# Score products that alternate between upper and lower rows, and r*k on GpSimd, in a linear-attention and two-MoE kernel

## Chip, cores and metric

One core of one Trainium2 chip. The metric is the device time of one execution in microseconds (us), lower is better. The engines are called TensorE (PE in the profile; PEld are its weight loads), VectorE (DVE), ScalarE (ACT), GpSimd (POOL) and SyncE (SP, which issues most DMAs). All tensors here are float32.

## The reference

The first of three layers is the one that the change touches: a linear attention with a per-element decay w, for 4 batches, 8 heads, 768 positions and heads of 48.

```
for t in range(S):
    cur = u * k_t (outer) v_t
    y[t] = r_t @ (state + cur)
    state = w_t * state + k_t (outer) v_t
```

Its output, as 3072 rows of 384, goes through a mixture of 8 experts with one expert per row (cosine logits, softmax gate, ReLU MLP 384-1024-384), and then through a second mixture in which each expert takes at most 384 rows, chosen greedily by score. These two layers are untouched.

## The kernel before, in words

The attention runs in 24 chunks of 128 positions (`NT = 24`), six to a batch (`C = 6`), all 8 heads of a chunk at once. The heads lie in pairs: head 2a in the lower 64 partitions and head 2a+1 in the upper 64 of block a, for a = 0 to 3 (`PR = 4`, `HP = 64`). Each engine has its own loop over the iterations t, and handles chunks at fixed distances from t; semaphores tie the loops together. One iteration moves every chunk on by one step.

- **VectorE**, iteration t: `take_x(t-1)` (L717), which adds the diagonal term to y; the two scans of the decays of chunk t+2, `scan_after` (L663) and `scan_before` (L673), with a small reciprocal (L666) between; `mask_scores(t+1)` (two instructions, L698); `add_state(t)` (L707, or L710 where t is a multiple of 6; none where t+1 is); `decay_k(t+2)` (L682), k times decay; `product(t+2)` (L690), r times k; and in two iterations of three some five tiny routing instructions (`choose`, `place`). `take_x` adds a term from SBUF to one from PSUM, and the mask is the only SBUF input of L698; the scans, L682 and L690 read two SBUF inputs each.
- **GpSimd**, iteration t: `decay_r(t+2)` (L467), r times decay, which waits for `scan_before(t+2)`, and from iteration 6 on `scatter(t-6)` (L478), an indirect DMA of finished rows.
- **ScalarE**, iteration t, in this order: `check(t+1)` (L507), `diag_evac(t+1)` (L539), `x_evac(t-1)` (L527), four heads of `weigh_v(t)` (L518), `y_evac(t)` (L533), `diag_out(t+1)` (L545), the other four heads, `k_evac(t+1)` (L554), `carry(t)` (L575), and in every third iteration `tokens` (L583).
- **TensorE**, iteration t: `score(t+1)` (L822), `diag_sums(t+1)` (L855), `update(t)` (L888), `x_forward(t-1)` (L829), `diag_back(t+1)` (L861), `values(t)` (L842 for the carried state, L846), `logits(t-1)` (L874), sometimes `counts`, `k_transposes(t+1)` (L918), `x_back(t)` (L926). Where t+1 is a multiple of 6 less one, that is in iterations 4, 10, 16 and 22, `scored` (L901) stands in the place of `k_transposes`, and the iteration after it has `scored_back` (L909) in the place of `update`. Where t is a multiple of 6 there is no L842.
- **SyncE** loads the chunk t+3 (`load_decays`) into one of three buffers as soon as `s_kdec`, `s_rdec` and `s_rk` say that chunk t has been read.

`score(t)` makes, for each pair a, two products of 64 rows of contraction, 128 columns of weights and 128 of moving data: one from the lower rows into the PSUM bank `p_g[0]`, one from the upper rows into `p_g[1]`. Each product in float32 is two weight loads and two matmuls, 16 of each per chunk. Before, all four of the lower rows are issued, then all four of the upper rows. In `values` the loop over h goes from one half to the other at every step, and has done so already. `product(t)` fills `rk[t % 2]`, which `diag_sums(t)` reads; `diag_back` needs ScalarE's copy of these sums.

The chain from one iteration to the next on ScalarE is written by these waits: `y_evac(t)` waits for the last product of `values(t)`; `diag_back(t+2)` waits for `diag_evac(t+2)`, which stands behind `diag_out`, `weigh_v`, `k_evac`, `carry` and `check` on ScalarE; `values(t+1)` is behind `diag_back(t+2)` on TensorE. `scan_after(t+2)` waits for `carry(t-1)`. `score(t+1)` waits for `decay_k(t+1)` and `decay_r(t+1)`.

Of the kernel before, what the change touches and what calls it, by code (L numbers as in the profile page):

```python
# [9 lines left out]
ALU = mybir.AluOpType  # L10
# [9 lines left out]
PR = H // 2  # L20
HP = 64
# [51 lines left out]
DB = 3  # L73
# [122 lines left out]
def attention(nc, general, sb, ps, sem, io, keep):  # L196
# [13 lines left out]
    kr_t = sb("kr_t", [P, DB, 2, PR, P], F32)  # L210
# [13 lines left out]
    rk = sb("rk", [P, 2, PR, P], F32)  # L224
# [42 lines left out]
    s_kr = [sem(f"s_lkr{i}", False) for i in range(DB)]  # L267
# [6 lines left out]
    s_rk = sem("s_rk")  # L274
    s_g = sem("s_g")
    s_masked = sem("s_masked")
# [8 lines left out]
    s_dsum = sem("s_dsum")  # L285
# [20 lines left out]
    def slot(t):  # L306
        return t % (RB * G)
# [5 lines left out]
    def flag(eng):  # L313
        eng.wait_ge(s_narrow, 4)
        return eng.value_load(bad[0:1, 0:1], min_val=0, max_val=1)
# [15 lines left out]
    with nc.Block() as block:  # L331
# [75 lines left out]
        def _(pool):  # L407
# [40 lines left out]
            def later_constants():  # L448
                pool.wait_ge(s_const, 25)
                const(pool.memset(keep["logits"][:, :, :], NEG))  # L450
                const(pool.memset(keep["tokens"][:, :], 0.0))
                pool.wait_ge(s_const, 27)

            def scores_of_first():

                pool.wait_ge(s_scored_out, 4)
                const(pool.tensor_copy(keep["w2s"][:, :, :, HD:HD + E],
                                       w2g[:, :, 0:2, :].rearrange("p m e o -> p e m o")))
                pool.wait_ge(s_const, 28)

            def decay_r(t):
                q = t % DB
                pool.wait_ge(s_kr[q], 16 * (t // DB + 1))
                pool.wait_ge(s_before, t + 1)
                if t >= 3:
                    pool.wait_ge(s_y, t - 2)
                pool.tensor_tensor(r_dec[:, t % 3, :, :], kr_t[:, q, 1, :, :], before[:, t % 2, :, 0:P],  # L467
                                   ALU.mult).then_inc(s_rdec, 1)

            def scatter(t):  # L470
                j = JOB_OF[t]
                if t == 0:
                    pool.wait_ge(s_clear, 16)
                pool.wait_ge(s_place, PLACE * (j + 1))
                pool.wait_ge(s_x, t + 1)
                pool.wait_ge(s_lgc, j + 1)
                pool.wait_ge(s_tok, j + 1)
                pool.indirect_dma_start(  # L478
                    out=sorted_rows[:, :],
                    out_offset=bass.IndirectOffsetOnAxis(ap=pos[:, slot(t):slot(t) + 1], axis=0),  # L480
                    in_=rows[:, slot(t), :], in_offset=None).then_inc(s_sc[slot(t)], 16)

            for t in range(-2, NT + G + 3):
                if t + 2 < NT:
                    decay_r(t + 2)
                if t == -1:
                    later_constants()
                if t == 3 * C - 2:
                    scores_of_first()
                if t - G - 3 == NT - 1:  # L490
                    bad_w = flag(pool)
                if t >= G + 3:
                    scatter(t - G - 3)
# [132 lines left out]
        def _(dve):  # L626
# [29 lines left out]
            def scan_after(t):  # L656
                q = t % DB
                dve.wait_ge(s_w[q], 16 * (t // DB + 1))
                if t >= 2:
                    dve.wait_ge(s_check, t - 1)  # L660
                if t >= 3:
                    dve.wait_ge(s_state, updates_before(t - 2))
                dve.tensor_tensor_scan(flat(after[:, t % 2, :, :])[:, ::-1], flat(w_pad[:, q, :, :])[:, ::-1],  # L663
                                       flat(last[:, :, :])[:, ::-1], 0.0, ALU.mult, ALU.add).then_inc(s_after, 1)
                dve.wait_ge(s_after, t + 1)
                dve.reciprocal(start[:, :, 0], after[:, t % 2, :, 1]).then_inc(s_inv, 1)  # L666

            def scan_before(t):
                q = t % DB
                dve.wait_ge(s_inv, t + 1)  # L670
                if t >= 2:
                    dve.wait_ge(s_rdec, t - 1)
                dve.tensor_tensor_scan(flat(before[:, t % 2, :, :]), flat(w_pad[:, q, :, :]), flat(start[:, :, :]),  # L673
                                       0.0, ALU.mult, ALU.add).then_inc(s_before, 1)
# [8 lines left out]
                                  ALU.mult).then_inc(s_kdec, 1)  # L683

            def product(t):
                q = t % DB
                dve.wait_ge(s_kr[q], 16 * (t // DB + 1))
                if t >= 2:
                    dve.wait_ge(s_dsum, t - 1)
                dve.tensor_tensor(rk[:, t % 2, :, :], kr_t[:, q, 0, :, :], kr_t[:, q, 1, :, :], ALU.mult  # L690
                                  ).then_inc(s_rk, 1)

            def mask_scores(t):
                for g in range(2):
                    dve.wait_ge(s_g, 2 * t + g + 1)
                    if t >= 2:
                        dve.wait_ge(s_y, t - 1)
                    dve.tensor_tensor(scores[:, t % 2, g, :, :], p_g[g][:, :, :],  # L698
                                      mask[:, :].unsqueeze(1).broadcast_to([P, PR, P]), ALU.mult).then_inc(s_masked, 1)
# [12 lines left out]
            def take_x(t):  # L712
                dve.wait_ge(s_yb, t + 1)
                dve.wait_ge(s_dv, t + 1)
                if t >= RB * G:
                    dve.wait_ge(s_sc[slot(t)], 16 * (t // (RB * G)))
                dve.tensor_tensor(rows[:, slot(t), 0:HD].rearrange("p (a h d) -> p a h d", a=PR, h=2),  # L717
                                  p_x[:, :, :].rearrange("p a (h d) -> p a h d", h=2)[:, :, :, 0:D],
                                  diag_v[:, t % 2, :, :].rearrange("p (a h) d -> p a h d", h=2), ALU.add
                                  ).then_inc(s_x, 1)  # L720
# [51 lines left out]
            for t in range(-2, NT + 3):  # L772
                if 0 <= t - 1 < NT:
                    take_x(t - 1)
                if t + 2 < NT:
                    scan_after(t + 2)
                    scan_before(t + 2)
                if t == 1:
                    dve.wait_ge(s_eT, 1)
                    dve.tensor_copy(enT[:, :, :], p_e).then_inc(s_en, 1)  # L780
                if t == -1:
                    dve.wait_ge(s_shape, 2)
                    dve.wait_ge(s_const, 24)
                if 0 <= t + 1 < NT:
                    mask_scores(t + 1)
                if 0 <= t < NT and t % C < C - 1:
                    add_state(t)
                if t + 2 < NT:
                    decay_k(t + 2)
                    product(t + 2)  # L790
                if t == 0:
                    normalize()
                if t == NT:
                    choose(LAST - 1)
                    place(LAST - 1)
                    judge()
                    dve.wait_ge(s_redo, AHEAD)
                    plan_redo(dve, keep, s_redo, AHEAD)
                for j, job in enumerate(JOBS):
                    if t == job[-1] + 1:  # L800
                        take_logits(j)
                    if t == job[-1] + 2 and j != LAST - 1:
                        choose(j)
                    if j == LAST and t == job[-1] + 2:
                        dve.wait_ge(s_narrow, 3)
                        dve.tensor_scalar(bad[:, :], p_d[:, 0, 0:1], float(P), None, ALU.is_lt).then_inc(s_narrow, 1)
                    if t == job[-1] + 3 and j != LAST - 1:
                        place(j)
# [4 lines left out]
        def _(pe):  # L813
            def score(t):
                pe.wait_ge(s_kdec, t + 1)
                pe.wait_ge(s_rdec, t + 1)
                for g in range(2):
                    half = slice(HP * g, HP * g + HP)
                    if t > 0:
                        pe.wait_ge(s_masked, 2 * (t - 1) + g + 1)  # L820
                    for a in range(PR):
                        ins = pe.matmul(p_g[g][:, a, :], k_dec[half, t % 2, a, :], r_dec[half, t % 3, a, :],  # L822
                                        start=True, stop=True)
                    ins.then_inc(s_g, 1)

            def x_forward(t):
                pe.wait_ge(s_x, t + 1)
# [141 lines left out]
            for t in range(-1, NT):  # L969
# [11 lines left out]
                if t == 1:  # L981
                    pe.wait_ge(s_norm, 10)
                    for a in range(KD):
                        ins = pe.transpose(p_e[:, a, :], emb[:, a * P:(a + 1) * P], ident[0:E, 0:E])
# [1505 lines left out]
```

## Time and profile before

| | us |
|---|---|
| median of 3 runs | 833.84 (833.01 to 835.03) |
| the profiled execution, whole | 829.33 |
| its span, first to last instruction | 827.5 |
| the attention's iterations 0 to 22 (by L861) | from 19.8 to 176.3 |

The span is the time between the program's first and last instruction in the profile; the execution's own time is 1.8 us more. A row of the timeline gives the start, the duration of a merged run of equal instructions, the engine, the line of the kernel, the operation with output and inputs, the count, and in brackets the idle time before it with what ended it. A run's duration goes from the start of its first instruction to the end of its last. "issue" means that nothing in the profile was waited for.

### The profile page before, as it was taken

To read this page: it belongs to the slowest core of one execution; us is meant where nothing else is said; L and a number is where in the kernel's file an instruction comes from. 1 tells how busy PE (TensorE), PEld (TensorE's weight loads), DVE (VectorE), ACT (ScalarE), POOL (GpSimd) and SP (SyncE) were. 2 spreads that over 40 slices of the span, in tenths; PEclk is the share of its full clock that TensorE was granted. 3 is DMA by queue.
4 is the path that set the end of the run, shared out by engine and by line. 5 is a ranking of instruction groups with operands and counts; after the bars stand their busy time and mean duration, and the time that the engine had idled before them with its cause. 6 is when DMAs were issued, how large, how long until landed. Compare 5 with 4: busy or idle time off the path is not lost. (4 is left out here: it accounts for less than half of the span.)

```text
span 827.5 us, 17288 instructions
## 1 busy us (share of the span) xinstructions
PE 790.9 (96%) x6003; PEld 577.1 (70%) x6004; DVE 438.1 (53%) x1194; ACT 323.3 (39%) x818; POOL 148.7 (18%) x151
## 2 busy tenths in 40 slices
PE   8999999997999999999999983999999999999996
PEld 7878787875788777778888762756565565665653
DVE  7889898955333333233233327666857686673000
ACT  3878786873444444444444440111121211112120
POOL 4113333322000000000000000105242230402201
PEclk9999999999999999999999995899999999999998
DMA  8869899813676657576575530513415051436100
GB/s 286 287 225 332 308 342 317 297 51 134 219 259 223 232 176 262 191 251 202 208 255 189 184 112 1 181 65 138 171 49 181 30 190 63 158 139 234 48 10 31
DMA packets 68850, 149.63 MB, mean 181 GB/s; under 512 B 4968, under 2 KB 37104, under 8 KB 68784
## 3 DMA queue, kind: packets, MB, share of 16 engines
q1 hardware_dynamic: 53952, 114.03, 39.3%
q0 software_dynamic: 6912, 23.75, 8.4%
q10 hardware_dynamic: 7920, 10.99, 4.1%
q8 instruction: 39, 0.64, 0.3%
q14 instruction: 27, 0.22, 0.1%
HBM read 130.06 MB, written 18.69 MB: 180 GB/s over the span
## 5 line engine op out<-in xcount | busy, mean ns | idle before, releaser
L1497 PE MATMUL p_o<-w2s,hid_t 128*128 (+1 forms) x432 | 152.7, 497 | 0.0
L1486 PEld LDWEIGHTS p_h<-x_t,w1s 128*128 128x128 f32 x1248 | 143.4, 192 | 7.2
L1486 PE MATMUL p_h<-x_t,w1s 128*128 128x128 f32 x1248 | 143.5, 275 | 0.0
L1970 PE MATMUL p_gh<-g_t,w1s 128*128 128x384 f32 x384 | 132.7, 494 | 0.0
L1986 PE MATMUL p_go<-w2s,g_hid 128*128 128x384 f32 x384 | 131.5, 489 | 0.0
L1497 PEld LDWEIGHTS p_o<-w2s,hid_t 128*128 128x128 f32 x432 | 78.7, 192 | 46.3 <-issue 1.8
L1970 PEld LDWEIGHTS p_gh<-g_t,w1s 128*128 128x128 f32 x384 | 70.0, 190 | 45.7 <-issue 6.1
L1986 PEld LDWEIGHTS p_go<-w2s,g_hid 128*128 128x128 f32 x384 | 70.3, 190 | 42.1
L1370 ACT ACTIVATE hid_t<-p_h 128x512 f32<-128x512 f32 x52 | 31.1, 597 | 155.3 <-PE p_h L1486 146.4
L1709 ACT ACTIVATE g_hid<-p_gh 128x384 f32<-128x384 f32 x64 | 31.4, 491 | 112.8 <-PE p_gh L1970 112.8
L1670 POOL DMA_INDIRECT g_in<-y_rows,table x24 | 29.6, 1233 | 244.5 <-DVE table L1829 239.6
L1423 DVE TENSOR_SCALAR col<-col 128x1 f32<-128x1 f32 x27 | 4.2, 154 | 131.0 <-ACT ex L1374 131.0
L1759 DVE TENSOR_TENSOR reach<-free_best,cand 128x3968 bf16<-128x3968 f32 (+2 forms) x19 | 58.6, 3082 | 0.7
L1680 POOL DMA_INDIRECT out<-o_row,table x24 | 43.8, 1825 | 79.7 <-ACT o_row L1702 44.8
L467 POOL TENSOR_TENSOR r_dec<-kr_t,decays 128x512 f32<-128x512 f32 x24 | 28.8, 1198 | 112.6 <-issue 65.4
L518 ACT ACTIVATE diag_v<-v_pad,diag 128x48 f32<-128x48 f32 x192 | 48.0, 327 | 0.0
L1702 ACT ACTIVATE o_row<-p_go 128x384 f32<-128x384 f32 x24 | 11.8, 491 | 87.7 <-PE p_go L1986 87.7
L822 PE MATMUL p_g<-r_dec,k_dec 64*128 64x128 f32 x384 | 41.0, 285 | 1.3 <-DMA u_blk<-in_u_blk 1.3
L822 PEld LDWEIGHTS p_g<-r_dec,k_dec 64*128 64x128 f32 x384 | 36.4, 187 | 5.2 <-issue 3.7
L1695 ACT ACTIVATE g_t<-p_gx 128x384 f32<-128x384 f32 x22 | 10.8, 491 | 71.3 <-PE p_gx L1957 71.3
L1374 ACT ACT_TABLE_LOAD x27 | 34.6, 1283 | 3.7 <-issue 3.2
L663 DVE TENSOR_TENSOR_SCAN decays<-w_pad,last 128x520 f32<-128x520 f32 x24 | 29.9, 1244 | 11.6 <-ACT state L575 9.3
(269 smaller groups left out, 1044.4 us busy)
## 6 DMA issues: line engine op xcount, KB each, us to landing
w1s<-in_w SPq DMA_DIRECT2D x28, 1536.0 KB, 6.5
kr_t<-in_kr_t SPq DMA_DIRECT2D x24, 512.0 KB, 5.3
w2t<-in_w_t SPq DMA_DIRECT2D x16, 768.0 KB, 7.5
w1s<-in_w1b SPq DMA_DIRECT2D x8, 1536.0 KB, 6.5
w2s<-in_w2b SPq DMA_DIRECT2D x8, 1536.0 KB, 10.1
w2s<-in_w POOLq DMA_DIRECT2D x12, 768.0 KB, 6.5
w_pad<-in_w_t SPq DMA_DIRECT2D x24, 256.0 KB, 5.8
v_pad<-in_v_pad SPq DMA_DIRECT2D x24, 256.0 KB, 7.5
```

What stands on the lines that cost most here:

```text
L518: ins = act.activation(diag_v[:, t % 2, h, :], v_pad[:, q, h, 0:D], ACT.Copy, scale=diag[:, t % 2, h:h + 1])
L663: dve.tensor_tensor_scan(flat(after[:, t % 2, :, :])[:, ::-1], flat(w_pad[:, q, :, :])[:, ::-1], flat(last[:, :, :])[:, ::-1], 0.0, ALU.mu ...
L822: ins = pe.matmul(p_g[g][:, a, :], k_dec[half, t % 2, a, :], r_dec[half, t % 3, a, :], start=True, stop=True)
L1370: act.activation(hid_t[:, half * g:half * (g + 1), :], p_h[g][:, :, :], ACT.Relu).then_inc(s_relu, 1)
L1374: act.activation(ex[:, :], lg[:, q, :], ACT.Exp, bias=col[:, q, 9:10], accum_out=col[:, q, 10:11]).then_inc(s_exp, 1)
L1486: ins = pe.matmul(p_h[g][:, m, :], w1s[:, q, a, f:f + P], x_t[:, q, a, :], start=(a == 0), stop=(a == KD - 1))
L1497: ins = pe.matmul(p_o[:, :], hid_t[:, m, :], w2s[:, bass.ds(half, 1), m, :].rearrange("p o n -> p (o n)"), start=(m == 0), stop=(m == KF - 1))
L1680: pool.indirect_dma_start(out=io["out"][:, :], out_offset=place(1, p, i), in_=o_row[:, p % 2, i, :], in_offset=None).then_inc(s_out[p % 2] ...
L1709: act.activation(hid[:, m, :], p_h[(KF * p + m) % 3][:, :], ACT.Relu).then_inc(s_relu, 1)
L1759: dve.tensor_tensor(reach(n)[:, at, :], free(p)[:, at].unsqueeze(2).broadcast_to([P, len(part), n]), cand[:, 0:n].unsqueeze(1).broadcast_t ...
L1970: ins = pe.matmul(p_h[n % 3][:, :], w1s[:, p % 2, a, m * P:(m + 1) * P], x_t[:, a, :], start=(a == 0), stop=(a == KD - 1))
L1986: ins = pe.matmul(p_o[n % 2][:, :], hid[:, m, i * P:(i + 1) * P], w2s[:, p % 2, m, 0:HD], start=(m == 0), stop=(m == KF - 1))
```

## The change

Three edits. `score` issues, for each pair a, the product of the lower rows and then that of the upper rows, and waits once for both masks of the chunk before, where it waited for each half's by itself; both signals now come at the end. GpSimd gets a `product` of its own, called ahead of `decay_r` for chunks 3 to 23. VectorE makes only chunks 0 to 2.

```
@@ gpsimd
+            def product(t):
+                q = t % DB
+                pool.wait_ge(s_kr[q], 16 * (t // DB + 1))
+                pool.wait_ge(s_dsum, t - 1)
+                if t == DB:
+                    pool.wait_ge(s_rk, DB)
+                pool.tensor_tensor(rk[:, t % 2, :, :], kr_t[:, q, 0, :, :], kr_t[:, q, 1, :, :], ALU.mult
+                                   ).then_inc(s_rk, 1)
...
             for t in range(-2, NT + G + 3):
                 if t + 2 < NT:
+                    if t + 2 >= DB:
+                        product(t + 2)
                     decay_r(t + 2)
@@ vector
                     decay_k(t + 2)
-                    product(t + 2)
+                    if t + 2 < DB:
+                        product(t + 2)
@@ tensor
             def score(t):
                 pe.wait_ge(s_kdec, t + 1)
                 pe.wait_ge(s_rdec, t + 1)
-                for g in range(2):
-                    half = slice(HP * g, HP * g + HP)
-                    if t > 0:
-                        pe.wait_ge(s_masked, 2 * (t - 1) + g + 1)
-                    for a in range(PR):
+                if t > 0:
+                    pe.wait_ge(s_masked, 2 * t)
+                for a in range(PR):
+                    for g in range(2):
+                        half = slice(HP * g, HP * g + HP)
                         ins = pe.matmul(p_g[g][:, a, :], k_dec[half, t % 2, a, :], r_dec[half, t % 3, a, :],
                                         start=True, stop=True)
-                    ins.then_inc(s_g, 1)
+                        if a == PR - 1:
+                            ins.then_inc(s_g, 1)
```

## Rows read from the trace of the kernel before

**Rows 1.** Windows, iterations 11 to 17: us, PE, PEld, DVE, ACT, POOL busy; clock, DMA, GB/s.

```profile
98.96:142.19 43.23, 43.23 (x552) 35.03 (x551) 38.10 (x76) 33.00 (x113) 15.51 (x13) 1.00 0.92 322
```

**Rows 2.** Costs by line, 0 to 200 us; after the bar busy us, mean ns.

```profile
L822 PE MATMUL p_g<-r_dec,k_dec 64*128 64x128 f32 x384 | 41.0, 285 | 1.3 <-DMA u_blk<-in_u_blk 1.3
...
L842 PE MATMUL p_y<-r_dec,state 64*64 64x128 f32 x320 | 21.8, 275 | 0.0
...
L690 DVE TENSOR_TENSOR rk<-kr_t 128x512 f32<-128x512 f32 x24 | 17.4, 723 | 0.0
```

**Rows 3.** Timeline, PE iterations 8 to 10: start us, duration us, instructions.

```profile
81.20 1.24 DVE L663 TENSOR_TENSOR_SCAN decays<-w_pad,last 128x520 f32<-128x520 f32 x1 [0.20 <-ACT state L575]
...
82.90 0.27 PE L861 MATMUL p_diag<-ident,diag_t 128*128 128x128 f32 x1
...
84.08 1.19 POOL L467 TENSOR_TENSOR r_dec<-kr_t,decays 128x512 f32<-128x512 f32 x1 [4.18 <-issue]
...
85.27 0.60 ACT L533 ACTIVATE y_tr<-p_y 128x512 f32<-128x512 f32 x1 [0.78 <-PE p_y L846]
85.29 0.68 DVE L682 TENSOR_TENSOR k_dec<-kr_t,decays 128x512 f32<-128x512 f32 x1
85.43 1.43 POOL L478 DMA_INDIRECT sorted_rows<-rows,pos  x1 [0.16 <-PE p_y L846]
...
86.31 0.60 PE L926 MATMUL p_x<-ident,y_tr 128*128 128x128 f32 x4
...
86.84 1.71 PE L822 MATMUL p_g<-r_dec,k_dec 64*128 64x128 f32 x16
...
87.20 1.00 ACT L575 ACTIVATE state<-state_sum,decays 128x48 f32<-128x48 f32 x4
...
88.33 1.24 DVE L663 TENSOR_TENSOR_SCAN decays<-w_pad,last 128x520 f32<-128x520 f32 x1 [0.82 <-ACT state L575]
...
89.25 0.26 ACT L539 ACTIVATE diag_t<-p_diag 128x128 f32<-128x128 f32 x1
...
89.84 0.27 PE L861 MATMUL p_diag<-ident,diag_t 128*128 128x128 f32 x1
```

**Rows 4.** Timeline of iterations 1 and 2, ScalarE's copies.

```profile
28.17 0.60 ACT L533 ACTIVATE y_tr<-p_y 128x512 f32<-128x512 f32 x1 [1.18 <-PE p_y L846]
...
32.05 0.26 ACT L539 ACTIVATE diag_t<-p_diag 128x128 f32<-128x128 f32 x1
```

**Rows 5.** Timeline of the start: lock between VectorE and GpSimd, and a wait on ScalarE.

```profile
7.23 1.47 POOL L467 TENSOR_TENSOR r_dec<-kr_t,decays 128x512 f32<-128x512 f32 x1 [1.09 <-DVE decays L673]
...
7.57 1.68 DVE L690 TENSOR_TENSOR rk<-kr_t 128x512 f32<-128x512 f32 x1
...
12.52 0.25 ACT L539 ACTIVATE diag_t<-p_diag 128x128 f32<-128x128 f32 x1
...
12.82 0.47 PE L861 MATMUL p_diag<-ident,diag_t 128*128 128x128 f32 x1 [1.31 <-ACT diag_t L539]
```

**Rows 6.** Timeline, iteration 11, then iteration 13.

```profile
97.32 1.24 DVE L663 TENSOR_TENSOR_SCAN decays<-w_pad,last 128x520 f32<-128x520 f32 x1 [0.51 <-ACT state L575]
...
98.96 0.27 PE L861 MATMUL p_diag<-ident,diag_t 128*128 128x128 f32 x1
...
100.20 1.19 POOL L467 TENSOR_TENSOR r_dec<-kr_t,decays 128x512 f32<-128x512 f32 x1 [6.22 <-issue]
101.15 0.79 DVE L682 TENSOR_TENSOR k_dec<-kr_t,decays 128x512 f32<-128x512 f32 x1
...
112.03 0.27 PE L861 MATMUL p_diag<-ident,diag_t 128*128 128x128 f32 x1
```

**Rows 7.** Timeline: GpSimd's back-to-back starts.

```profile
134.44 1.18 POOL L467 TENSOR_TENSOR r_dec<-kr_t,decays 128x512 f32<-128x512 f32 x1 [4.35 <-issue]
...
135.57 0.28 POOL L457 COPY w2s<-w2g 128x128 f32<-128x128 f32 x1
...
174.88 0.96 POOL L478 DMA_INDIRECT sorted_rows<-rows,pos  x1 [0.30 <-issue]
```

## The prediction

> **What bounds the kernel now.** I read the windows by stage first, then the timeline of one iteration, then the costs by line. In the windows: the stretch of one batch, six iterations from one L861 to the sixth after it: 43.23 us long, TensorE busy for all 43.23, VectorE for 38.10, ScalarE 33.00, GpSimd 15.51, at a granted clock of 1.00 [rows 1]. TensorE never waits for data here; it is the bound, at 6.94 us for an ordinary iteration (82.90 to 89.84) [rows 3], 9.12 where the iteration holds `scored` (89.84 to 98.96) and 13.07 for the next two together (98.96 to 112.03) [rows 3, 6]. But VectorE has only 5 us of slack in 43, and ScalarE, with 10, sits in a chain with TensorE. So I ask of each of the other engines: when TensorE gets quicker, which loop of waits closes next, and how long is it?
>
> **Part 1, `score` in turns.** 16 matmuls of L822 last 1.71 us [rows 3], and L842, also 16 with 64 rows and 128 moving columns, lasts 21.8/20 = 1.09 us [rows 2]. L842 already changes halves at every step. One 128-column float32 matmul follows another in the same rows after (0.60 - 0.27)/3 = 0.11 us (L926) [rows 3]. 16 in single file would need 15 x 0.11 + 0.27 = 1.92; the old order gets 1.71, as lower and upper meet for a moment at the change. In turns they go as eight pairs: 7 x 0.11, 0.10 more after the first (a run that starts cold), and 0.27 for the last: 1.15 us, **0.56 us less, so TensorE's own iteration falls to 6.38**. The single wait for both masks costs nothing: `score(t+1)` waits for `decay_k(t+1)`, which VectorE issues behind `mask_scores(t)`. That both signals now come at the end costs nothing either: the score of 86.84 ends at 88.55, and VectorE, which starts the first of two scans of 1.24 at 88.33 [rows 3], comes to the masks after 90.8. The first chunks differ, but save 0.5 us as a whole.
>
> **Part 2, what catches TensorE: ScalarE's loop.** From `diag_back` to `y_evac` 2.37 us (82.90 to 85.27) [rows 3]; from there to `diag_evac` of the next iteration ScalarE works without a break, 3.88 us (28.17 to 32.05) [rows 4], 3.98 with `tokens` (85.27 to 89.25) [rows 3]; from `diag_evac` to a `diag_back` that waited for it 0.30 (12.52 to 12.82) [rows 5]. The sum is 6.55, or 6.65 with `tokens`. That is below today's 6.94, so it is hidden now, and above 6.38: of the 0.56 us only 0.3 to 0.4 can come out in an ordinary iteration. With nothing else in the way a batch would take about 41 us, 2.2 less, and the attention 8.4 less.
>
> **Part 3, `product` off VectorE.** It takes 0.72 us there [rows 2], (17.4 - 1.68)/23 = 0.68 without one long case [rows 5]. VectorE's loop goes over two iterations: `carry` ends at 88.20, `scan_after` starts 0.13 later; from it to the end of `decay_k` 4.77 (81.20 to 85.97) [rows 3]; 0.06 to `score`; `score` to L861 3.00 now (86.84 to 89.84), 2.44 then; 2.37 to `y_evac`; 2.93 to the end of `carry` (85.27 to 88.20). Together 12.70 for two iterations, 6.35 each: product, which stands behind `decay_k`, was not in it. Its removal alone therefore gives no time; it gives 0.5 us of slack in two iterations.
>
> **Part 4, `product` on GpSimd.** Price: the same operation with the same shape, 1.19 us [rows 3]. GpSimd is idle for 4 us in each iteration (the bracket of the row at 84.08), so by busy time it is free. But it shares something with VectorE: at the start VectorE's product, which began 1.13 us before GpSimd's r_dec was over, took 1.68 us, not 0.68 [rows 5], and `decay_k`, begun 0.24 before r_dec's end, took 0.79 instead of 0.68 [rows 6]. Both read two SBUF operands, as the scans do. So the one that comes second waits for the end of the first, and gets back 0.13 us of it. Where does the new product lie?
> - Chunks 4 to 8, no scatter yet: right behind r_dec. A small GpSimd operation behind r_dec began 0.05 before its end [rows 7]; `decay_k` begins 1.21 after r_dec's start [rows 3], so product, at 1.14, is first, and `decay_k` waits some 1.0 us. VectorE's loop becomes 13.7, 6.85 each: nearly nothing is gained there.
> - Chunks 9 to 23: behind the scatter. `scan_after` to r_dec 2.88 (81.20 to 84.08), r_dec to the end of the scatter 2.78 (84.08 to 86.86) [rows 3], a gap, product 1.19, and then the next `scan_after`, which gets back 0.13. The gap is not in the trace: 0.05 us of overlap behind r_dec and 0.30 between two scatters [rows 7] bound it; I take the middle, 0.10. **GpSimd's loop: 2.88 + 2.78 + 0.10 + 1.19 - 0.13 = 6.82.** It closes because `scan_after` would be ready 2.37 + 2.93 + 0.13 = 5.43 after the last L861, while product runs (from 4.6 to 5.8, if the scan before began at 5.43 - 6.55 = -1.12). This loop is longer than ScalarE's, so it sets the ordinary iteration.
>
> The Trainium skill (SBUF — State Buffer, Who interferes with whom) says that the second of the two "fully blocks" until the first is done. By full blocking the loop would be 6.95 and the whole would gain 3.8 us in the place of 5.3; the two rows above speak for the 0.13.
>
> The scatter stays at 1.43: it began while `decay_k` ran and 0.96 is its length alone [rows 3, 7]; `decay_k` stays where it is. `load_decays` waits for `s_rk`, which now comes before `s_kdec`; the load goes out no later. Product waits for `diag_sums` of two chunks before, which TensorE made an iteration earlier.
>
> **The sum.** L861 of iteration 11 is 0. `scan_after` is at -1.64 now (97.32) [rows 6], -1.1 when L861 comes 0.5 sooner. GpSimd's loop of 6.82 lets the next one start at 5.7, at 5.5 as `decay_k` has no add_state ahead of it here and lets the scatter go 0.2 earlier. Then 4.77 to the end of `decay_k`, 0.06 and 2.44: L861 of 13 is at 12.78 (13.07 now). Three iterations at 6.82 follow (43.23 - 13.07 - 9.12 = 21.04 together now), then the one with `scored`: 9.12 less 0.5, as `check` on ScalarE holds `diag_evac` a little, 8.61. A batch: 12.78 + 20.46 + 8.61 = 41.85 against 43.23, **1.4 us less**.
> - Start to iteration 5: 0.5 at the first chunks, 0.3 over iterations 2 to 4, 0.5 at `scored`: 1.3.
> - Iterations 5 to 11: product is free in the first two of these, 0.6 there instead of 0.3: 1.7.
> - Iterations 11 to 17: 1.4. Iterations 17 to 22: 0.3 + 0.6 = 0.9.
>
> Total **5.3 us**. Behind it nothing moves: routing and both expert layers start earlier by as much. The profiled execution of 829.33 would become 824.0, its span 822.2. The median of the runs is 4.5 above that execution, and I take the difference from the median: **828.5**.
>
> **Rivals.**
> - *ScalarE's loop alone* (GpSimd's gap is -0.05, or product and scatter are shorter): 6.67 for GpSimd's loop, then 6.55 for ScalarE's. Gain 7 to 8.4: 826. For it: all its terms are rows. Against: it needs GpSimd to be better than the middle.
> - *GpSimd's loop is longer*: gap 0.30, some 15 iterations times 0.2 less: gain 2.3, 831.5. For it: two scatters are 0.30 apart.
> - *The pairs don't overlap*, as 128 columns of weights are loaded where L842 loads 64, and the change does nothing for TensorE. Then 6.94 stays, and GpSimd's 6.82 hides below it: 833.8. Against: the old order's 1.71 is below 1.92 already.
> - *Slower: product on GpSimd is much longer than 1.19.* r_dec took 1.47 when it ran into VectorE's work [rows 5]. Product starts while scans are near; if it waits behind one, or shares its reads, GpSimd's loop grows one for one. From 1.4 us the loop passes 7.0, today's mean of the three iterations that it sets (21.04/3); from 1.9 the kernel is slower by more than 0.2%; at 2.1, the loop is 7.73 and a batch 13.7 + 23.2 + 8.6 = 45.5, 2.3 more than now; 5.5 in the chunks from 7 on, less 1.3 of the start: 838. Against: GpSimd gets there first in my schedule, as `scan_after` waits for `carry`.
>
> The Trainium skill (GPSIMD Engine Reference, Performance versus the Vector engine) speaks against elementwise work on GpSimd, by a factor of about two. Here it is 1.19 to 0.68; the loss is not in that factor but in whom the queue holds up.
>
> **How the numbers follow.** Forecast 0.50; ScalarE's loop alone 0.18; longer loop of GpSimd 0.17; pairs don't overlap 0.06; product long, slower 0.09. 0.2% is 1.7 us, about what a measurement of this kernel can tell from no change. Faster: 0.50 + 0.18 and 0.12 of the 0.17, 0.80. Same: the 0.05 left of it, the 0.06, and 0.01 of the last, 0.12. Slower 0.08. The range goes from 825.0 (the second case's end) to 832.5 (the third with 1 us more).
>
> **What the next profile would show.** L822 x16 at 1.15 us; if 1.7, part 1 is wrong. L539 ahead of each L861, or L663 starting at the end of a GpSimd product: whichever stands there is the new bound. `decay_k` (L682) near 1.7 us in chunks 3 to 7, 0.68 later. GpSimd's product at 1.19. L861 to L861 at 6.8, and TensorE with idle time ahead of L861 or L822. If L861 to L861 is 6.4, a wait that I call binding is not there; if it is over 7.0, the fourth rival holds. And the layers behind must keep their length; if they change, the sum is wrong in a place where I looked for nothing.

## The result, and the profile after

Forecast: 5.3 us faster. Measured: **slower**. Median 836.57 us (835.1 to 837.85, 13 runs) against 833.56 (831.7 to 836.17, 13 runs); ratio 1.0032, interval 1.0021 to 1.0042: 0.32%, or 2.7 us, more. That is over the 0.2% that can be told from no change, and above the forecast's range (825.0 to 832.5).

The lines that answer to [rows 2]. `score` is now L835, `product` on GpSimd L476; L674 and L684 are the scans, L693 `decay_k`, L875 `diag_back`. The view is the costs by line, 0 to 205 us, of the changed kernel.

```profile
L674 DVE TENSOR_TENSOR_SCAN decays<-w_pad,last 128x520 f32<-128x520 f32 x24 | 36.1, 1504 | 5.1 <-ACT state L586 3.0 <-DMA w_pad<-in_w_t 2.0
...
L835 PE MATMUL p_g<-r_dec,k_dec 64*128 64x128 f32 x384 | 28.0, 285 | 9.5 <-DVE k_dec L693 7.5 <-DMA u_blk<-in_u_blk 1.8
L476 POOL TENSOR_TENSOR rk<-kr_t 128x512 f32<-128x512 f32 x21 | 27.7, 1318 | 4.0 <-DVE rk L702 3.6
...
L693 DVE TENSOR_TENSOR k_dec<-kr_t,decays 128x512 f32<-128x512 f32 x24 | 21.5, 894 | 0.0
...
L752 DVE SCALAR_TENSOR_TENSOR c_at_best<-c_at_best,rank_of 128x24 f32<-128x24 f32 (+2 forms) x9 | 10.3, 1142 | 0.3
...
L782 DVE CAST pos<-pos_f 128x3 uint32<-128x3 f32 (+2 forms) x9 | 8.0, 886 | 0.3
```

`score` went from 41.0 to 28.0 us: 1.16 each, as forecast. But its idle time, 1.3 us before, is 9.5, and `decay_k` on VectorE is what it waits for. The first scan has a mean of 1504 ns in the place of 1244. And two rows stand high in this list that were at the very end of the old one: L752, a routing step on 24 elements per partition, has a mean of 1142 ns, where it took 180, and the cast L782, which took 174, has 886. These means mix three shapes; in the batch shown below, the two L752 have a mean of 1921 ns and the two casts 1472.

The same by stretch: one batch, from the L875 of iteration 11 to that of iteration 17 (windows; columns as in [rows 1]).

```profile
99.60:143.66 44.06, 40.46 (x553) 31.78 (x551) 42.45 (x70) 33.03 (x113) 23.40 (x19) 1.00 0.92 317
179.08:204.73 25.65, 19.22 (x199) 15.05 (x198) 7.69 (x45) 10.09 (x34) 6.66 (x7) 1.00 0.24 82
```

44.06 us against 43.23 [rows 1]. TensorE, which was busy for all of the stretch, is now idle for 3.6 of it. VectorE does less work (no r*k, 4.1 us per batch) and is busy for longer, 42.45 against 38.10. So its instructions hold 42.45 - (38.10 - 4.1) = 8.45 us of waiting inside their own durations: **1.4 us per chunk**. The timeline from VectorE's iteration 7 shows one such wait.

```profile
72.59 0.68 DVE L693 TENSOR_TENSOR k_dec<-kr_t,decays 128x512 f32<-128x512 f32 x1
72.71 1.45 POOL L487 DMA_INDIRECT sorted_rows<-rows,pos  x1 [0.15 <-issue]
...
73.33 1.16 PE L835 MATMUL p_g<-r_dec,k_dec 64*128 64x128 f32 x16 [0.60 <-DVE k_dec L693]
73.39 0.18 DVE L751 TENSOR_TENSOR c_at_best<-rows,c_best 128x24 f32<-128x24 f32 x1
73.61 1.90 DVE L752 SCALAR_TENSOR_TENSOR c_at_best<-c_at_best,rank_of 128x24 f32<-128x24 f32 x1
...
74.18 1.28 POOL L476 TENSOR_TENSOR rk<-kr_t 128x512 f32<-128x512 f32 x1
...
75.55 0.18 DVE L755 TENSOR_REDUCE c_first_best<-c_at_best 128x3 f32<-128x24 f32 x1
```

L752 has two operands in SBUF. It began at 73.61 and ended at 75.51, 0.05 after GpSimd's product (74.18 to 75.46). It began 0.57 us *ahead* of that product, when GpSimd was still in its scatter; 0.18 us should have seen it through. The next iteration, in the same view:

```profile
81.85 1.49 DVE L782 CAST pos<-pos_f 128x3 uint32<-128x3 f32 x1
82.01 1.29 POOL L476 TENSOR_TENSOR rk<-kr_t 128x512 f32<-128x512 f32 x1
...
83.25 0.54 DVE L729 TENSOR_TENSOR rows<-p_x,diag_v 128x384 f32<-128x384 f32 x1
83.72 1.22 DVE L674 TENSOR_TENSOR_SCAN decays<-w_pad,last 128x520 f32<-128x520 f32 x1
...
83.85 0.33 PE L843 MATMUL p_x<-ident,rows 128*128 128x128 f32 x1 [0.57 <-DVE rows L729]
```

There it is the cast L782, begun 0.16 ahead of the product, and `take_x` and the scan behind it are late; TensorE's `x_forward` waits 0.57 for `take_x`. In the third iteration of each three, without routing steps at this place, it is the scan L674 (2.1 to 2.9 us):

```profile
111.02 2.74 DVE L674 TENSOR_TENSOR_SCAN decays<-w_pad,last 128x520 f32<-128x520 f32 x1
111.36 1.30 POOL L476 TENSOR_TENSOR rk<-kr_t 128x512 f32<-128x512 f32 x1
```

The three kinds of wait sum up to the 8.4 us of the batch: 3.5 at L752, 2.6 at the cast, 2.3 at the scan.

Where the loss lies, by the starts of L861 before and L875 after: iteration 5 at 55.73 and 55.38, 11 at 98.96 and 99.60, 17 at 142.19 and 143.66, 22 at 176.29 and 179.08. So it is 0.4 ahead at first, then loses 1.0, 0.8 and 1.3. From there to the end of this stretch, the first output product of the expert layer, it takes 25.65 us (179.08 to 204.73) and took 24.15 (176.29 to 200.44). That part has no changed instruction, its length also varies among the experiments' traces, and why stays open.

### The profile page after: what moved, and what is told of

Its sections match the earlier page's. It is cut to its first block and busy times, and to the rows that moved or that the text cites. A ratio compares the mean times of both kernels' runs of the same rounds, so it can differ in the third digit from the quotient of the medians.

```text
span 836.1 us, 17288 instructions
## 1 busy us (share of the span) xinstructions
PE 782.5 (94%) x6003; PEld 566.9 (68%) x6004; DVE 453.5 (54%) x1173; ACT 323.3 (39%) x818; POOL 174.1 (21%) x172
## 5 line engine op out<-in xcount | busy, mean ns | idle before, releaser
L1694 POOL DMA_INDIRECT out<-o_row,table x24 | 40.6, 1693 | 78.1 <-ACT o_row L1716 44.8
L674 DVE TENSOR_TENSOR_SCAN decays<-w_pad,last 128x520 f32<-128x520 f32 x24 | 36.1, 1504 | 5.1 <-ACT state L586 3.0
L835 PE MATMUL p_g<-r_dec,k_dec 64*128 64x128 f32 x384 | 28.0, 285 | 9.5 <-DVE k_dec L693 7.5
```

What stands on the lines that cost most here:

```text
L1694: pool.indirect_dma_start(out=io["out"][:, :], out_offset=place(1, p, i), in_=o_row[:, p % 2, i, :], in_offset=None).then_inc(s_out[p % 2] ...
```

## The experiments

Chips differ: the kernel before has a median of 834.45 beside the first four runs and of about 828 beside the others. So times are compared by their ratio to the kernel before on the same chip, and mechanisms by the length of a batch from iteration 11 to 17 in the traces. The microseconds in the expectations of runs 5 to 8 were written with a kernel before of about 834 us in mind; on that chip's scale their ratios of 0.9973, 0.9857, 0.9967 and 0.9888 are 832, 822.5, 831.7 and 825 us. A trace is one execution, and what it shows for iterations 0 to 22 is within some 3 us of the gain in the medians, no closer. Line numbers shift a little from kernel to kernel.

**1 to 4. Each half alone, and what it is about GpSimd's work.**

```
# e1: the order of score, r*k left on VectorE
# e2: r*k on GpSimd, the old score
# e3 = e1, and on GpSimd in the place of product(t + 2), into a tile that nobody reads:
+                pool.tensor_tensor(spare[:, t % 2, :, :], kr_t[:, q, 0, :, :], kr_t[:, q, 1, :, :], ALU.mult)
# e4 = e1, and there:
+                pool.memset(spare[:, 0, :, :], 0.0)
+                pool.memset(spare[:, 1, :, :], 0.0)
```

> Only the order in score changes; r*k stays on VectorE. Lock theory (GpSimd's product keeps VectorE's two-operand and casting instructions waiting, and that alone makes the change slower): without it the gain of score stays. The iteration is then held by ScalarE's loop at 6.55 to 6.65 us and by VectorE's own work in the iterations with routing (4.77 + 0.60 + 0.96 + 0.50 = 6.8), a batch takes 41.0 to 41.8 us in the place of 43.2, and the kernel 826 to 829 us, 5 to 8 below before. Rival (the single wait for both masks, or the two signals that come together at the end, hold VectorE up): this kernel is slower than before as well, about 836, with L698 waiting for L822.

> Only r*k moves to GpSimd; score is issued in the old order. Lock theory: VectorE is the bound with or without the quicker score, at 44.06 us per batch, so this takes the same 836 to 837.5 us as the whole change, with the same long instructions (scan L674 over 2 us in one chunk of three, the routing's SCALAR_TENSOR_TENSOR 1.9 us, CAST 1.5 us). Rival (score is at fault): within 1 us of before.

> The new score order, r*k on VectorE as before, and on GpSimd an additional product of the same operands into a spare tile, at the place where the change has its product. Nothing needs its result. Lock theory: VectorE is held as in the whole change (1.4 us per chunk) and makes r*k besides (0.68): a batch takes about 44.1 + 6 x 0.68 = 48.1 us, the kernel 850 to 856. Rival (it is GpSimd's queue that comes late with r_dec): VectorE's instructions keep their lengths, and the time is that of the whole change or less, at most 837.

> As the one before, but the additional GpSimd work is two memsets of 128x512 into the spare tile, which read nothing (about 1.0 us together by the 0.47 us of the memset of 396 columns in the trace of before). Lock theory: what counts is that both sides read a second operand from SBUF; VectorE's scans and routing keep 1.24 and 0.18 us and the time is that of the new score order alone, within 1 us; a CAST may still be held. Rival (occupied queue of GpSimd): the same loss as with the additional product.

| | ratio to before (interval) | median us |
|---|---|---|
| score order alone | 0.9898 (0.9880 to 0.9915) | 826.03 |
| r*k on GpSimd alone | 1.0075 (1.0058 to 1.0092) | 840.12 |
| score order, extra product on GpSimd | 1.0091 (1.0070 to 1.0111) | 841.54 |
| score order, extra memsets on GpSimd | 0.9895 (0.9875 to 0.9915) | 825.87 |

The windows of one batch, iterations 11 to 17, of the score order alone:

```profile
94.67:136.11 41.44, 40.67 (x553) 31.87 (x551) 37.84 (x76) 32.90 (x113) 15.56 (x13) 1.00 0.95 327
```

of r*k on GpSimd alone:

```profile
100.69:145.91 45.22, 43.58 (x553) 35.03 (x551) 42.65 (x70) 33.37 (x113) 23.35 (x19) 1.00 0.90 310
```

of the extra product:

```profile
99.59:145.34 45.75, 41.98 (x552) 33.05 (x551) 44.75 (x76) 33.17 (x113) 23.37 (x19) 0.96 0.89 302
```

and of the extra memsets:

```profile
95.55:136.84 41.29, 40.59 (x552) 31.84 (x551) 37.83 (x76) 32.81 (x113) 21.64 (x25) 1.00 0.94 329
```

So the change has two halves of opposite sign. The new order of `score` gives 1.8 us per batch and 1.0% of the time; the single mask wait and the late signals cost nothing that can be seen. r*k on GpSimd costs 2.0 us per batch with the old order (45.22 against 43.23) and 2.6 with the new one (44.06 against 41.44). That it takes more time by itself (1.0075) than in the whole change (1.0032) I had not expected. VectorE is busy for as long in both (42.65 and 42.45) but idle for 2.6 us of the batch, not 1.6. My reading is that VectorE's loop of waits leads through `score`, so the quicker score helps VectorE too; no run isolates this.

Extra product against extra memsets is the pair that tells what it is. Both fill GpSimd's queue at the same place, 7.8 and 6.5 us per batch. With memsets VectorE is busy for 37.83 us, with the product for 44.75: 1.15 us per chunk. A row of the costs by line over the batch, of the extra product:

```profile
L754 DVE TENSOR_TENSOR c_at_best<-rows,c_best 128x24 f32<-128x24 f32 x2 | 3.1, 1536 | 0.1
L775 DVE TENSOR_TENSOR slot_pick<-slot_of,chosen 128x24 f32<-128x24 f32 x2 | 3.0, 1524 | 0.1
...
L785 DVE CAST pos<-pos_f 128x3 uint32<-128x3 f32 x2 | 0.3, 169 | 0.1
```

and of the extra memsets:

```profile
L785 DVE CAST pos<-pos_f 128x3 uint32<-128x3 f32 x2 | 1.1, 568 | 0.1
...
L775 DVE TENSOR_TENSOR slot_pick<-slot_of,chosen 128x24 f32<-128x24 f32 x2 | 0.4, 182 | 0.1
...
L754 DVE TENSOR_TENSOR c_at_best<-rows,c_best 128x24 f32<-128x24 f32 x2 | 0.4, 182 | 0.1
```

The two-operand routing steps take 1.5 us beside the product and 0.18 beside the memsets. Only the cast L785 is a little longer beside memsets, 0.57. So the queue is not what costs; it is GpSimd's reading. TensorE's granted clock of 0.96 in this window (0.79 in the iteration from 107.02 to 115.27) isn't the cause of the 45.75 us: the batch before it, from 53.73 to 99.59, took 45.86 at a clock of 1.00. My size for the extra product (850 to 856) was too high: a batch took 45.75, not 48.1. Of the 2.4 us between them, 1.8 is VectorE, busy for 44.75 and not 42.45 + 4.1, and 0.6 is that it was idle for 1.0 and not 1.6.

**5. Reading one operand.**

```
# e5 = e1, and on GpSimd at the same place:
+                pool.tensor_copy(spare[:, t % 2, :, :], kr_t[:, q, 0, :, :])
```

> As with the additional product, but the additional GpSimd work is a copy of k (128x512) into the spare tile: it reads one operand from SBUF, where the product reads two and the memsets none. If any GpSimd instruction that reads SBUF keeps VectorE's two-operand instructions waiting, L663, L682, L739 or L760 get longer by the rest of the copy, some 0.7 us per chunk, a batch takes 42 to 44 us (41.3 with memsets, 45.8 with the product) and the kernel 829 to 835. If only two-operand reads do, it is 826, as with memsets.

Ratio 0.9973 (0.9954 to 0.9992). The batch:

```profile
94.35:137.26 42.91, 40.38 (x552) 31.79 (x550) 40.95 (x76) 33.08 (x113) 19.42 (x19) 1.00 0.94 322
```

A copy of 0.62 us costs VectorE (40.95 - 37.84)/6 = 0.5 us per chunk. One read operand is enough, and the cost, 0.5 us for a copy of 0.62 and 1.15 for a product of 1.30, goes with the length in these two.

**6. What bounds the new order of score.**

```
# e6: the order of score, r*k on VectorE, and on ScalarE:
                 if t + 1 < NT:
-                    check(t + 1)
                     diag_evac(t + 1)
+                    check(t + 1)
```

> The new score order alone, and on ScalarE diag_evac ahead of check. It takes 1.15 us out of ScalarE's loop (6.55 to 5.4). If that loop alone sets the 6.58 to 6.72 of the score order alone, the iterations fall to TensorE's 6.38, a batch to 40 us and the kernel to 820 to 822. If VectorE is as near (its iteration with routing is 4.77 + 0.60 + 0.96 + 0.50 = 6.8), a batch stays at 40.8 to 41.4 and the kernel within 2 us of 826.

**Ratio 0.9857 (0.9830 to 0.9883), 816.69 us: the fastest kernel of the study.**

```profile
90.88:131.61 40.73, 40.05 (x553) 31.74 (x551) 37.86 (x76) 32.73 (x114) 15.54 (x13) 1.00 0.96 334
```

0.7 us less per batch; two ordinary iterations of three came down to 6.38 to 6.42 (62.91 to 69.30, 103.61 to 110.00), which is TensorE's own length as worked out; the third, with `counts`, takes 6.61. So the iterations did what I expected of ScalarE's loop alone, while the batch of 40.73 lies between the 40 of that case and the 40.8 of the other. With the score order alone they stood at 6.57 (107.35 to 113.92) to 6.72, and its timeline shows ScalarE's loop closed:

```profile
75.02 0.60 ACT L533 ACTIVATE y_tr<-p_y 128x512 f32<-128x512 f32 x1 [1.02 <-PE p_y L847]
...
78.94 0.26 ACT L539 ACTIVATE diag_t<-p_diag 128x128 f32<-128x128 f32 x1
...
79.26 0.32 PE L862 MATMUL p_diag<-ident,diag_t 128*128 128x128 f32 x1
```

L862 (the old L861) of the iteration before is at 72.60: 2.42 us to `y_evac`, 3.92 from there to `diag_evac`, 0.32 to the next L862, together 6.66.

**7 and 8. Is it the engine or the place?**

```
# e7: the whole change, and on GpSimd
                     decay_r(t + 2)
+                    if t + 2 >= DB:
+                        product(t + 2)
# and on VectorE decay_k(t + 2) ahead of mask_scores(t + 1) and add_state(t)
# e8 = e7, and diag_evac ahead of check
```

> The whole change with two moves: VectorE makes k times decay ahead of the two masks, and GpSimd makes its product right behind r times decay, ahead of the scatter. Then r times decay and product (2.5 us) run beside the masks, add_state and take_x (2.2 us), none of which reads two SBUF operands. Theory (it is where the product lies, not that it is on GpSimd): VectorE loses at most 0.7 us for r times decay held by k times decay and some tenths in the iterations with routing; a batch takes 41.3 to 42.5 us, the kernel 826 to 831. Rival (r*k on GpSimd costs wherever it is): 835 or more.

> As the one before, and diag_evac ahead of check on ScalarE. With VectorE freed of the product (0.6 us per chunk) and ScalarE's loop at 5.4, TensorE's 6.38 would be the bound: a batch 40 to 40.8 us, the kernel 820 to 824. If the product still holds VectorE in the iterations with routing, it is not better than the order of score with diag_evac first.

Ratios 0.9967 (0.9944 to 0.9989) and 0.9888 (0.9862 to 0.9914). The batches, of the first:

```profile
94.93:137.18 42.25, 40.84 (x552) 31.93 (x550) 36.86 (x70) 32.92 (x113) 22.77 (x19) 1.00 0.94 327
```

and of the second:

```profile
92.51:133.18 40.67, 40.02 (x553) 31.77 (x551) 36.73 (x70) 32.84 (x114) 22.77 (x19) 1.00 0.98 340
```

With r*k on GpSimd in both, VectorE is busy for 36.86 and 36.73 us, less than with r*k on it (37.84), though not by the whole 4.1 of r*k: some 0.5 us of waiting per chunk is left. The timeline of the first shows why. The one that waits is now also GpSimd: r times decay, begun while `decay_k` runs, takes 1.48 us and not 1.19. The product stands beside the mask, which has one operand in SBUF, and `add_state`, which has one; of the routing steps L772, and in another iteration L751, still wait, 0.77 in the place of 0.18.

```profile
116.65 0.67 DVE L693 TENSOR_TENSOR k_dec<-kr_t,decays 128x512 f32<-128x512 f32 x1
...
116.88 1.48 POOL L467 TENSOR_TENSOR r_dec<-kr_t,decays 128x512 f32<-128x512 f32 x1 [3.67 <-issue]
117.23 1.28 DVE L710 TENSOR_TENSOR scores<-p_g,mask 128x512 f32<-128x512 f32 x2
...
118.33 1.30 POOL L476 TENSOR_TENSOR rk<-kr_t 128x512 f32<-128x512 f32 x1
...
118.43 0.35 DVE L719 TENSOR_TENSOR state_sum<-p_u,state 128x192 f32<-128x192 f32 x1
...
118.90 0.77 DVE L772 TENSOR_TENSOR slot_pick<-slot_of,chosen 128x24 f32<-128x24 f32 x1
```

It is the place. But it isn't better than leaving r*k on VectorE: with `diag_evac` first TensorE's 6.39 is reached in both (batches of 40.67 and 40.73), and the medians on the same chip are 818.53 and 816.69. Without it the batch is longer than with the score order alone (42.25 against 41.44), for a reason apart from VectorE: the scatter now comes behind the product, and `tokens` on ScalarE waits 0.71 us for it at 107.00, ahead of `check` and `diag_evac`; that iteration takes 6.88 us. In the batch before, where `tokens` doesn't wait, it is 6.03, and that batch takes 41.37 us (41.30 with the score order alone).

**9 to 11. Who bounds the changed kernel; when does the wait begin; a control.**

```
# e9: the whole change, and diag_evac ahead of check
# e10: the whole change, and in GpSimd's product, ahead of the tensor_tensor:
+                pool.memset(fence[:, :], 0.0).then_inc(s_fence, 1)
+                pool.wait_ge(s_fence, t - DB + 1)
# e11: the kernel before, and diag_evac ahead of check
```

> The whole change, and diag_evac ahead of check on ScalarE, which took 0.6 us out of every batch of the score order alone (41.3 to 40.7). If VectorE with its waits is the bound of the changed kernel, a batch stays within 0.5 us of 44.06 and the time within 0.3% of the whole change. Rival (ScalarE's loop still has a part in it): 43.4 or less.

> The whole change with a memset of one column on GpSimd ahead of its product, and a wait for it, so that the product is only issued when the scatter before it is done. In the changed kernel SCALAR_TENSOR_TENSOR (L752) started at 73.61 and the scan L674 at 111.02, 0.57 and 0.34 us ahead of the product's recorded start and while the scatter still ran, and both waited to the product's end. If the product takes the shared port when it is issued, behind the running scatter, the fence shortens each such wait: L752 runs through in 0.18 us where it started ahead, and the longest scans lose 0.3 to 0.6 us; a batch takes 42.8 to 43.8. If the recorded start of the product is only late in the profile, nothing changes but 0.1 to 0.2 us per chunk for the fence: 44 to 45.

> The kernel before, with diag_evac ahead of check and nothing else. TensorE is busy for all of a batch's 43.23 us there, and ScalarE's loop of 6.55 lies below its 6.94: no change, batch 43.2, time within 0.2% of before. If it gains as it does on top of the new score order, ScalarE's loop was no matter of that order.

The first: ratio 1.0024 (1.0011 to 1.0038), batch 44.02. ScalarE's loop has no part that can be seen in the changed kernel's batch. The control: batch 43.22, with TensorE busy for all of it, as before; its ratio of 0.9981 (0.9965 to 0.9996) is less than 0.2% and lies outside the batches. The second was the surprise: **ratio 0.9966 (0.9950 to 0.9983), faster than before**, for a memset of one column and a wait.

```profile
96.48:138.33 41.85, 40.44 (x552) 31.82 (x550) 38.03 (x70) 32.86 (x113) 25.71 (x25) 1.00 0.96 334
```

VectorE is busy for 38.03 us instead of 42.45, the batch takes 41.85 instead of 44.06. I had expected a smaller gain (42.8 to 43.8): right in direction, too small in size. The timeline of VectorE's iteration 10 in this kernel (L754 to L762 are the routing steps, L480 the product):

```profile
91.17 1.46 POOL L491 DMA_INDIRECT sorted_rows<-rows,pos  x1
...
91.87 0.18 DVE L755 TENSOR_TENSOR c_at_best<-rows,c_best 128x24 f32<-128x24 f32 x1
92.08 0.18 DVE L756 SCALAR_TENSOR_TENSOR c_at_best<-c_at_best,rank_of 128x24 f32<-128x24 f32 x1
...
92.51 0.18 DVE L762 TENSOR_TENSOR chosen<-c_at_best,c_first_best 128x24 bf16<-128x24 f32 x1
...
92.63 0.12 POOL L478 MEMSET fence<- 128x1 f32 x1
92.83 1.30 POOL L480 TENSOR_TENSOR rk<-kr_t 128x512 f32<-128x512 f32 x1
```

L756, which was L752, is through in 0.18 us beside the same scatter. Without the fence the product, already issued and with its own waits met, held VectorE's second operand from some point within the scatter on: after 73.57, when L751 ended normally, and no later than 73.79, when L752 should have ended. The recorded start is 74.18. (Whether the lock is taken so early, or the record of GpSimd's start is late by as much, no run tells apart; VectorE's time is the same either way.) With the fence it can't be issued before the scatter is done. The Trainium skill (GPSIMD Engine Reference, Instruction dispatch) says that each of GpSimd's cores starts the next instruction as soon as it has finished its share of this one, and that a wait on the earlier one's completion semaphore keeps the two in order. The two traces agree with it; that single cores were ahead is shown by neither.

The fence also shifts whom the product meets. No routing step and no cast of the batch waits any more (0.18 and 0.17 us), but the scans still do, about 3.7 us together, and in two of six iterations the product itself waits behind a scan and takes 1.98 to 2.21 us. From 86 us on:

```profile
86.27 1.24 DVE L678 TENSOR_TENSOR_SCAN decays<-w_pad,last 128x520 f32<-128x520 f32 x1 [0.35 <-ACT state L590]
86.44 2.16 POOL L480 TENSOR_TENSOR rk<-kr_t 128x512 f32<-128x512 f32 x1
...
87.76 1.94 DVE L688 TENSOR_TENSOR_SCAN decays<-w_pad,start 128x520 f32<-128x520 f32 x1
```

How much of the gain is the earlier start of the wait and how much the new order of arrival, this run doesn't divide. And the kernel is still slower than the score order alone (ratios 0.9966 and 0.9898).

## Why the prediction was wrong, point by point

- **Part 1, score in turns: right.** 1.16 us against 1.15, and TensorE's iteration 6.39 against 6.38, once nothing else bound. No cost of the single wait can be seen.
- **Part 2, ScalarE's loop: right.** 6.55 to 6.65 forecast, 6.57 to 6.72 measured with the score order alone; a batch 41.44 against "about 41". The gain of that kernel was 8.4 us, the very figure of this part, and that is luck: a batch gained 1.8 and not 2.2, and iterations 0 to 22 take 150.1 us in its trace against 156.5, 6.5 less. Moving `diag_evac` took the bound away.
- **Part 3, r*k off VectorE gives nothing by itself: not contradicted, but not tested alone.** The kernels with and without it on VectorE reach the same 40.7 per batch; another engine is the bound in both. The sum that leaves product out of VectorE's loop holds only where `scan_after` waits for `carry`. In the kernel before, the scans at 60.61, 74.24, 103.88 and 117.46, behind routing steps, have no such wait; there VectorE runs through, with product in the chain.
- **Part 4 is the step that failed**: GpSimd's loop of 6.82 us, in which only `scan_after` meets the product. For the batch the sum had 12.78 us for iterations 12 and 13, 20.46 for the next three and 8.61 for the last; the changed kernel has 13.35, 22.08 and 8.63. It failed in two ways. *First, the beginning of the wait.* I let `product` hold VectorE from its recorded start, "from 4.6 to 5.8" after L861. It holds it from within the scatter on, up to 0.57 us earlier. With the fence a batch takes 2.2 us less, 41.85 in the place of 44.06. That this is the sum's figure to the digit is luck: the six iterations are 12.98, 20.25 and 8.62, of the three in the middle two take 6.57 and 6.67, ScalarE's loop, and one 7.01, and product took 1.30 us or about 2, never 1.19. *Second, who is held.* I named the scans and `decay_k` as the instructions with two operands in SBUF, and the loops have no term at all for the routing steps beside the product. L739, L740, L746 and L760 read two operands as well, and the cast L770 is held with one. A step of 24 elements waits as long as a scan: 1.9 us. In two iterations of three one of them takes the whole wait, which the table of the old costs can't show, as nothing of GpSimd that reads SBUF lay beside them. The fence takes away both ways at once, so its 2.2 us are for the two together.
- *The early chunks* came as said: product's start 0.05 ahead of r_dec's end (28.62 against 27.48 + 1.19), `decay_k` 1.68 to 1.78 us ("near 1.7").
- *The price of product*, 1.19 by r times decay, was 1.30 where it ran unhindered.
- *"The second gets back 0.13 us"*: right for `decay_k` (0.68 + 29.92 - 28.80 = 1.80 by a full wait, 1.68 measured). It holds for the others too: L752 ended 0.13 sooner than a full wait and its 0.18 would give (75.46 + 0.18 - 75.51), the scan at 111.02 0.14 sooner. So full blocking, the case of 6.95, isn't what was missing. (The two sensitivities also count differently: 0.2 us was taken 15 times, 0.13 us only some 12 times for its 1.5.)
- *The rival that came nearest* is "slower: product waits behind a scan or shares its reads", which I gave 0.09. It had the sign, and GpSimd's loop over 7.0 as its test (it was (135.03 - 112.95)/3 = 7.36 from iteration 13 to 16), but its mechanism was a longer product. In the changed kernel product keeps its 1.30, and it was VectorE's own instructions that grew; so an iteration over 7.0 didn't tell the two apart, as the list of signs had it. A product that waits behind a scan came only with the fence.
- *"Behind it nothing moves"*: not so in the two profiled executions. Their spans are 8.6 us apart (836.1 and 827.5), of which 2.8 are there at iteration 22 and 1.5 in the last routing, as above; the other 4.3 lie in the expert layers, which have no changed instruction. The medians are only 3.0 apart, so most of the 8.6 is what one execution differs from another, and the attention's 2.8 would make up nearly the whole of the medians' difference.

## What to carry to other kernels

Before an elementwise step is moved to GpSimd, list every VectorE instruction that may run beside it, the smallest too: each with two operands in SBUF, and each cast, can wait for the whole GpSimd instruction, so put the step beside work that reads PSUM. Where it stands behind an indirect DMA in GpSimd's queue, a one-column memset and a wait ahead of it kept it here from holding VectorE early. And when a change joins a gain and a move, time the halves: here one half alone was worth 1.0%, and with one more line, 1.4%.

## What was not expected of the hardware

- A GpSimd product of 1.30 us held VectorE for up to 1.90 - 0.18 = 1.7 us (L752) and 2.94 - 1.24 = 1.7 us (the longest scan), as it began to do so while the scatter ahead of it still stood in the trace.
- Of GpSimd's work, a product (two operands read) and a copy (one read) held VectorE's two-operand instructions; memsets, which read nothing, did not (37.83 us busy per batch against 37.84 without them). The cast of 3 elements is held by the product (1.47 us), and by memsets for 0.4 us.
- The scatter held none of the VectorE instructions seen beside it: L751 (the old L739) ran through in 0.18, and `decay_k` in 0.68. It is the scatter that is longer there, 1.45 us where it starts while `decay_k` runs and 1.01 in e7, where it starts behind it. The Trainium skill (SBUF — State Buffer, Who interferes with whom) says that a two-operand instruction of VectorE meets only GpSimd instructions that read SBUF, that casts can take both ports, and that the order of issue decides who waits; product, copy, memsets and cast agree, and the fence bears out the last.
